# An unrolled attention stage with q, k and v laid out by the host, and a gate on the split x

## The chip, the cores and the metric

The kernel runs on one core of a Trainium2 chip, in one launch. The metric is the device time of that launch in microseconds, lower is better. All times here are of the kernel before; "the profiled execution" is one more execution of it, taken by the hardware profiler. Engines: PE is TensorE (PEld are its weight loads, which run beside its matmuls), DVE is VectorE, ACT is ScalarE, POOL is GpSimd, SP is SyncE, which issues most of the DMAs.

## What is computed

The reference, cut to what matters:

```python
# attention inside chunks of 64 tokens; q, k, v are [4, 8, 576, 64]
scores = (q_c @ k_c.T) / 8;  scores -= scores.max(-1)
attn = exp(scores) / (exp(scores).sum(-1) + 1e-9)
out = attn @ v_c                       # x = out as [2304 tokens, 512]
# mixture of experts, 8 experts, 512 -> 1024 -> 512
logits = x @ w_gate;  P = exp(logits - logits.max())
for _ in range(8):                     # balancing over rows and columns
    P /= P.sum(1) + 1e-9;  P /= P.sum(0) + 1e-9;  P *= N / E
out = sum over e of P[:, e:e+1] * (maximum(x @ w1[e], 0) @ w2[e])
# a last layer 512 -> 2048 -> 512
g = elu(out @ w_in);  result = g @ w_out
```

## The kernel before, in words

The 2304 tokens are 18 tiles of 128, in 6 blocks of 3 tiles. The experts and the last layer are 20 passes of 512 hidden columns each: a pass multiplies every block "up" (four groups of 12 matmuls with 384 columns, in groups f of 0 to 3) and "down" (three tiles of 12 matmuls with 512 columns). Each float32 operand of a pass is split in a rounded part and a rest (`x_hi`/`x_lo`, `w_hi`/`w_lo`, `h_hi`/`h_lo`), and three of the four products are taken.

The attention stage (blocks 0 to 5) runs together with pass 0: while block i's three tiles go through attention, the passes' work on block i-1 fills PE's gaps. What fills them is cut in `UNITS`: "up" f in two halves of 6 matmuls (`up_half`, L308) and "down" j in two halves of 6 (`down_tile`, L335), 14 units a block. The order is the hand-written list `STAGES` (L43), read by `block_schedule` (L55), the same on all engines; blocks 2 to 4 are a hardware loop, the others are unrolled. After block 5 the units of block 5 come alone (L442), then pass 1 begins (L448).

A tile's attention has six steps. **S0**: PE turns q and k by 4 transposes each into `ab_ps` (L370, L375), and ACT copies q (L519) and half of k (L522) out, DVE the other half of k (L661), into `k_wide`, which keeps zeros beside each chunk of k. **S1**: 8 float32 matmuls give the scores of all heads (L385; the trace has two records for each float32 matmul), DVE takes the row maximum (L665) and subtracts it (L668), ACT takes the exponential in two halves of 64 partitions (L530). **S2**: 8 transposes, one a head (L399), copied out by ACT (L536) and DVE (L673). **S3**: 8 matmuls with the turned exponentials as stationary operand and the values, with a column of ones beside them, as moving operand of 65 columns (L407); DVE adds to the sums (L677), takes reciprocals (L679) and multiplies (L682) to get `x_row`. **S4**: 4 transposes of x (L413), copied out by DVE (L687); ACT rounds it to `x_hi` (L540). **S5**: 4 float32 matmuls with 8 columns for the gate (L420), DVE copies the logits (L690) and makes `x_lo` (L694).

SP loads q, k and v of a tile with two DMAs each (L248) as its buffers come free. ACT issues the first 2 MB of weights (L566, L567), and splits them piece by piece (L506) in the last gaps of block 0, DVE making the rests (L646). POOL fills constants at the start (L276 to L284), takes the maximum over partitions once (L287) and scales the sum once after pass 1 (L295). The matmuls of the later passes are at L317 to L360.

## Time and profile before

| | us |
|---|---|
| median of 3 runs (lowest, highest) | 2164.53 (2163.47, 2165.15) |
| the profiled execution, its own time | 2163.2 |
| its span, first to last instruction | 2161.4 |
| PE busy in the span | 2130.3 |
| DVE, ACT, POOL busy | 823.4, 455.9, 22.4 |
| start to the first "up" of pass 0 | 57.91 |
| start to the first matmul of pass 1 | 259.31 |

The span is read as three stretches: the first block's attention alone, then five blocks of attention with pass 0 woven in (184.6 us together), then everything from pass 1 on, which the change does not edit. The granted clock is the share of full speed (2.4 GHz) that TensorE was given, 0.5 being 1.2 GHz.

### The profile page before, as it was taken

Reading aid. Unit: us, or ns where it says so; the run is one execution under the profiler, and the core shown is the slowest. Engines: PE = TensorE matmul, PEld = TensorE weight load, DVE = VectorE, ACT = ScalarE, POOL = GpSimd, SP = SyncE. Lnnn points to the kernel's source line nnn. Section 1 sums busy time; section 2 is a strip of 40 time slices with the busy share of each in tenths; the row PEclk is TensorE's granted clock in tenths of the full one; section 3 lists DMA queues with packets and bytes.
Section 4 is the critical chain, followed back from the end, with each engine's and each line's share of the span. In section 5 each row is a group of like instructions: output and inputs, shape, how many; then the busy total and the mean of one; then the engine's idle time right before and its main releaser. Section 6 shows DMA issues by size and latency. Waiting matters only on the chain.

```text
span 2161.4 us, 30934 instructions
## 1 busy us (share of the span) xinstructions
PE 2130.3 (99%) x11248; PEld 1937.2 (90%) x11248; DVE 823.4 (38%) x1439; ACT 455.9 (21%) x882; POOL 22.4 (1%) x29
## 2 busy tenths in 40 slices
PE   6999999999999999999999999999999999999999
PEld 5888899999999999999999999999999989999998
DVE  3444443332333233333333332333233345555544
ACT  3333311111111111111111111111111133223222
POOL 0000003000000000000000000000000000000000
PEclk8999999999999999999999999999999999999999
DMA  5223100000000100000000001000000000000001
GB/s 126 60 59 97 40 20 20 20 20 20 19 19 19 39 19 19 19 19 19 19 19 19 19 19 35 23 19 19 19 19 19 19 20 20 20 20 20 0 30 58
DMA packets 81304, 61.39 MB, mean 28 GB/s; under 512 B 58480, under 2 KB 58480, under 8 KB 81264
## 3 DMA queue, kind: packets, MB, share of 16 engines
q1 hardware_dynamic: 79680, 58.73, 9.0%
q10 hardware_dynamic: 1584, 2.11, 0.3%
q8 instruction: 26, 0.43, 0.1%
q14 instruction: 14, 0.11, 0.0%
HBM read 56.12 MB, written 4.72 MB: 28 GB/s over the span
## 4 chain that ended last, share of the span: by engine, by line
PE 96%; DVE 2%; issue 1%; ACT 1%; DMA 0%; ACTq 0%; SPq 0%; DVEq 0%; POOL 0%; POOLq 0%
PE down_ps L360 29%; PE up_ps L327 22%; PE ab_ps L360 14%; PE ab_ps L327 11%; PE cd_ps L327 11%; PE down_ps L346 2%; PE cd_ps L407 2%; PE up_ps L317 2%; PE cd_ps L385 1%; PE ab_ps L399 1%; PE ab_ps L413 1%; DVE row_max L665 1%; DVE x_row L682 0%; DVE soft L668 0%; PE cd_ps L480 0%
## 5 line engine op out<-in xcount | busy, mean ns | idle before, releaser
L513 ACT ACTIVATE h_hi<-up_ps 128x384 fp32r<-128x384 f32 x204 | 100.4, 492 | 1002.9 <-PE up_ps L327 955.9
L770 DVE SCALAR_TENSOR_TENSOR acc<-down_ps,route,acc 128x512 f32 x168 | 123.9, 751 | 424.0 <-PE down_ps L360 418.4
L651 DVE SCALAR_TENSOR_TENSOR h_lo<-up_ps,h_hi 128x384 fp32r<-128x384 f32 x204 | 113.8, 558 | 301.3 <-ACT h_hi L513 301.3
L360 PE MATMUL down_ps<-w_hi_b,h_lo 128*128 128x512 f32 x480 | 187.7, 391 | 0.0
L360 PE MATMUL down_ps<-w_lo_b,h_hi 128*128 128x512 f32 x480 | 187.4, 390 | 0.0
L360 PE MATMUL down_ps<-w_hi_b,h_hi 128*128 128x512 f32 x480 | 186.9, 389 | 0.0
L360 PE MATMUL down_ps<-w_hi_a,h_lo 128*128 128x512 f32 x432 | 169.0, 391 | 0.0
L360 PE MATMUL down_ps<-w_hi_a,h_hi 128*128 128x512 f32 x432 | 169.0, 391 | 0.0
L360 PE MATMUL down_ps<-w_lo_a,h_hi 128*128 128x512 f32 x432 | 168.7, 391 | 0.0
L327 PE MATMUL up_ps<-x_hi,w_lo_b 128*128 x480 | 161.1, 336 | 0.0
L327 PE MATMUL up_ps<-x_hi,w_hi_b 128*128 x480 | 161.0, 335 | 0.0
L327 PE MATMUL up_ps<-x_lo,w_hi_b 128*128 x480 | 160.8, 335 | 0.0
L327 PE MATMUL up_ps<-x_hi,w_hi_a 128*128 (+1 forms) x432 | 145.0, 336 | 1.7 <-DVE x_lo L805 1.7
L327 PE MATMUL up_ps<-x_hi,w_lo_a 128*128 (+1 forms) x432 | 145.0, 336 | 0.0
L327 PE MATMUL up_ps<-x_lo,w_hi_a 128*128 (+1 forms) x432 | 144.7, 335 | 0.0
L360 PEld LDWEIGHTS down_ps<-w_hi_b,h_lo 128*128 128x128 f32 x480 | 90.1, 188 | 18.8
L360 PEld LDWEIGHTS down_ps<-w_hi_b,h_hi 128*128 128x128 f32 x480 | 90.1, 188 | 17.2
L360 PEld LDWEIGHTS down_ps<-w_lo_b,h_hi 128*128 128x128 f32 x480 | 90.1, 188 | 17.1
L651 DVE SCALAR_TENSOR_TENSOR h_lo<-cd_ps,h_hi 128x384 fp32r<-128x384 f32 x90 | 50.2, 558 | 136.0 <-ACT h_hi L513 136.0
L651 DVE SCALAR_TENSOR_TENSOR h_lo<-ab_ps,h_hi 128x384 fp32r<-128x384 f32 x90 | 50.2, 558 | 132.2 <-ACT h_hi L513 132.2
L360 PEld LDWEIGHTS down_ps<-w_hi_a,h_lo 128*128 128x128 f32 x432 | 81.1, 188 | 17.0
L360 PEld LDWEIGHTS down_ps<-w_hi_a,h_hi 128*128 128x128 f32 x432 | 81.2, 188 | 15.3
(144 smaller groups left out, 4279.9 us busy)
## 6 DMA issues: line engine op xcount, KB each, us to landing
stage<-in_moe_w SPq DMA_DIRECT2D x30, 1024.0 KB, 5.0
q_raw<-in_q SPq DMA_DIRECT2D x36, 128.0 KB, 2.4
k_raw<-in_k SPq DMA_DIRECT2D x36, 128.0 KB, 2.8
v_raw<-in_v SPq DMA_DIRECT2D x36, 128.0 KB, 2.9
out<-acc SPq DMA_DIRECT2D x18, 256.0 KB, 2.0
stage<-in_moe_w_in SPq DMA_DIRECT2D x4, 1024.0 KB, 5.0
stage<-in_moe_w_out SPq DMA_DIRECT2D x4, 1024.0 KB, 5.1
stage<-in_moe_w ACTq DMA_DIRECT2D x2, 1024.0 KB, 8.8
```

The source lines that it names most:

```text
L317: mm = nc.tensor.matmul(up_ps[f % 2][:, 0:BLK], *terms[n], start=n == 0, stop=n == len(terms) - 1)
L327: mm = nc.tensor.matmul(hid_ps[f], w, x, start=n == 0, stop=n == len(terms) - 1)
L346: mm = nc.tensor.matmul(down_ps[j % 2][:, :], h, w, start=f == 0 and n == 0, stop=f == FT - 1 and n == 2)
L360: mm = nc.tensor.matmul(y_ps[j], h, w, start=f == 0 and n == 0, stop=f == FT - 1 and n == 2)
L385: mm = nc.tensor.matmul(scores[cs, 2 * m:2 * m + 2, :], q_t[:, m, cs], k_wide[:, m, c, :, :], start=True, stop=True)
L399: mm = nc.tensor.transpose(ab_ps[:, g, m * P:(m + 1) * P], e_wide[:, EH * g + m, :], ident[:, :])
L407: mm = nc.tensor.matmul(attn[:, g, m, :], e_t[:, EH * g + m, :], v_raw[j][:, EH * g + m, :], start=True, stop=True)
L413: mm = nc.tensor.transpose(ab_ps[:, 0, m * P:(m + 1) * P], x_row[:, 2 * m:2 * m + 2, :], ident[:, :])
L513: nc.scalar.activation(h_hi[:, f, :], bank, ACT.Relu).then_inc(h_hi_done, 1)
L651: nc.vector.scalar_tensor_tensor(h_lo[:, f, :], bank, 0.0, h_hi[:, f, :].bitcast(F32), ALU.max, ALU.subtract).then_inc(h_lo_done, 1)
L665: nc.vector.tensor_reduce(row_max[:, :], scores, AX_X, ALU.max).then_inc(max_done, 1)
L770: nc.vector.scalar_tensor_tensor(acc_tile(t), y_ps[j], route_flat[:, bass.ds(EXPERTS * t + expert, 1)], acc_tile(t), ALU.mult, ALU.add).th ...
```

## The change

The kernel's inputs q, k and v are laid out by the host before the launch (outside the metric): q and k transposed, tile by tile, so that a tile's q is 128 x 512 with head pairs on partitions and k is 64-row halves, and v by chunk and head pair. The turns of q and k (S0) and their copies are gone; SP loads q with one DMA and k and v with two each, straight into `q_t`, `k_wide` and `v_wide`, three buffers of each. The zeros of `k_wide` and `v_wide` are written by DVE (12 memsets of 64 x 512; `zero`). The softmax is normalised before the values: after one full-width exponential in place, DVE sums the rows (a new reduce), adds, takes reciprocals and multiplies into `x_row`, and PE turns two heads at once (4 transposes a tile for 8). The values are the stationary operand now, 64 columns each, and the turned weights move, 64 columns at a time: 16 matmuls a tile that write x already transposed. So x needs no turn and no copy, and ACT and DVE read `x_hi` and `x_lo` from PSUM. The gate is made once a block, from `x_hi` and `x_lo` with a padded 128-column stationary `gate_wide` (rounded weights in columns 0 to 7, rests in 8 to 15), copied by ACT, turned back by 3 transposes and added by DVE. POOL makes the rests of the first weights in place of DVE. Everything in the stage is unrolled.

On every engine the order (here tiles 6 to 8; "up1.1a" is half a of up 1 of block 1) is:

```
scores6 max6 shift6 down0.1b values5 x_hi5 x_lo5 down0.2a norm6 down0.2b up1.0a turn6 up1.0b
scores7 max7 shift7 up1.1a values6 x_hi6 x_lo6 gate1 gate_copy1 up1.1b norm7 up1.2a up1.2b turn7 up1.3a
scores8 max8 shift8 up1.3b values7 x_hi7 x_lo7 gate_turn1 logits1 down1.0a norm8 down1.0b down1.1a turn8
```

After tile 17 come gate5, then the 14 units of block 5 with `gate_turn(5)` behind the second, DVE's maximum of the logits there and its wait for POOL's `all_max` behind the fourth. The diff, cut to its core (new functions of PE, ACT and DVE stand as they are; of the removed ones see the listing above):

```diff
+def attention_schedule():
+    units = iter([(what, b, n, h) for b in range(BLOCKS - 1) for what, n, h in UNITS])
+    def some(count):
+        return [next(units) for _ in range(count)]
+    out = [("scores", 0), ("max", 0), ("shift", 0), ("scores", 1), ("max", 1), ("norm", 0), ("shift", 1), ("turn", 0),
+           ("scores", 2), ("max", 2), ("norm", 1), ("shift", 2), ("values", 0), ("x_hi", 0), ("x_lo", 0), ("turn", 1),
+           ("weights", 0), ("norm", 2), ("values", 1), ("x_hi", 1), ("x_lo", 1), ("turn", 2)]
+    for t in range(TPB, TILES):
+        b, where = divmod(t, TPB)
+        out += [("scores", t), ("max", t), ("shift", t)]
+        out += some(0 if b == 1 and where == 0 else 1)
+        out += [("values", t - 1), ("x_hi", t - 1), ("x_lo", t - 1)]
+        if where == 0:
+            out += [("weights", 1)] if b == 1 else some(1)
+            out += [("norm", t)] + some(1 if b == 1 else 2)
+        elif where == 1:
+            out += [("gate", b - 1), ("gate_copy", b - 1)] + some(1) + [("norm", t)] + some(2)
         else:
+            out += [("gate_turn", b - 1), ("logits", b - 1)] + some(1) + [("norm", t)] + some(2)
+        out += [("turn", t)] + some(0 if where == 2 else 1)
+    out += some(1) + [("values", TILES - 1), ("x_hi", TILES - 1), ("x_lo", TILES - 1)] + some(2)
+    assert next(units, None) is None
...
+        q_t = [at_arena(f"q_t{j}", [P, PAIRS, P]) for j in range(TPB)]
+        k_wide = [at_arena(f"k_wide{j}", [P, PAIRS, 2, 2, CHUNK]) for j in range(TPB)]
+        v_wide = [at_arena(f"v_wide{j}", [P, PAIRS, 2, 2, HD]) for j in range(TPB)]
+        e_t = at_arena("e_t", [P, PAIRS, P])
...
+        gate_wide = nc.alloc_sbuf_tensor_at("gate_wide", [P, KT, P], F32R, offset=acc_at + 4 * D * (TILES - 3))
+        gate_rows = nc.alloc_sbuf_tensor_at("gate_rows", [2 * EXPERTS, BLK], F32, offset=acc_at + 4 * D * (TILES - 2))
...
+        e_ps = ab_ps[:, 0, :]
+        x_ps = cd_ps[:, 1, :].rearrange("p (m n) -> p m n", m=KT)
+        gate_ps = ab_ps[:, 1, 0:BLK]
+        logit_ps = ab_ps[:, 1, BLK:BLK + 2 * TPB * EXPERTS].rearrange("p (j a e) -> p j a e", j=TPB, a=2)
...
+            def load_tile(t):
+                j = t % TPB
+                if t >= TPB:
+                    sp.wait_ge(scores_done, t - TPB + 1)
+                sp.dma_start(q_t[j][:, :, :], q[t, :, :, :]).then_inc(qk_loaded[j], 16)
+                for g in range(2):
+                    half = slice(HD * g, HD * g + HD)
+                    sp.dma_start(k_wide[j][half, :, :, g, :], k[t, half, :, :, :]).then_inc(qk_loaded[j], 16)
+                if t >= TPB:
+                    sp.wait_ge(values_done, t - TPB + 1)
+                for g in range(2):
+                    half = slice(CHUNK * g, CHUNK * g + CHUNK)
+                    sp.dma_start(v_wide[j][half, :, :, g, :], v[t, half, :, :, :]).then_inc(v_loaded[j], 16)
+            for t in range(TILES):
+                load_tile(t)
...
-            nc.gpsimd.memset(v_all[:, :, :, HD:VD], 1.0).then_inc(raw_free, TPB)
             nc.gpsimd.memset(ident[:, :], 0.0).then_inc(ident_zero, 1)
-            nc.gpsimd.memset(ones[:, :], 1.0).then_inc(const_ready, 1)
             pool.wait_ge(ident_zero, 1)
             nc.gpsimd.affine_select(out=ident[:, :], in_=ident[:, :], compare_op=ALU.not_equal, fill=1.0, base=0,
                                     pattern=[[-1, P]], channel_multiplier=1).then_inc(const_ready, 1)
-            nc.gpsimd.memset(e_wide[:, :, :], 0.0).then_inc(const_ready, 1)
-            nc.gpsimd.memset(k_wide[:, :, :, :, :], 0.0).then_inc(const_ready, 1)
+            nc.gpsimd.memset(gate_wide[:, :, :].bitcast(F32), 0.0).then_inc(gate_zero, 1)
+            nc.gpsimd.memset(ones[:, :], 1.0).then_inc(const_ready, 1)
+            pool.wait_ge(gate_hi_done, 1)
+            nc.gpsimd.tensor_tensor(gate_wide[:, :, EXPERTS:2 * EXPERTS], gate_w[:, :, :],
+                                    gate_wide[:, :, 0:EXPERTS].bitcast(F32), ALU.subtract).then_inc(gate_lo_done, 1)
+            for n in range(PIECES):
+                layer, kk = divmod(n, KT)
+                pool.wait_ge(w_hi_done, n + 1)
+                nc.gpsimd.tensor_tensor(w_lo[0][:, layer, kk, :], stage[:, layer, kk, :],
+                                        w_hi[0][:, layer, kk, :].bitcast(F32), ALU.subtract).then_inc(w_lo_done, 1)
...
+            def gate_rows_of(b):
+                pe.wait_ge(x_lo_done, TPB * (b + 1))
+                if b == 0:
+                    pe.wait_ge(gate_lo_done, 1)
+                else:
+                    pe.wait_ge(logits_done, b)
+                cols = slice(BLK * b, BLK * (b + 1))
+                for kk in range(KT):
+                    for x in (x_hi, x_lo):
+                        mm = nc.tensor.matmul(gate_ps, gate_wide[:, kk, :], x[:, kk, cols],
+                                              start=kk == 0 and x is x_hi, stop=kk == KT - 1 and x is x_lo)
+                mm.then_inc(gate_done, 1)
+            def gate_turn(b):
+                pe.wait_ge(gate_rows_done, b + 1)
+                for j in range(TPB):
+                    at = BLK + 2 * EXPERTS * j
+                    mm = nc.tensor.transpose(ab_ps[:, 1, at:at + 2 * EXPERTS], gate_rows[:, P * j:P * j + P],
+                                             ident[0:2 * EXPERTS, 0:2 * EXPERTS])
+                mm.then_inc(gate_turned, 1)
+            def attention(what, t):
+                j, r = t % TPB, t // TPB
+                if what == "scores":
+                    pe.wait_ge(qk_loaded[j], 48 * (r + 1))
+                    if t < TPB:
+                        pe.wait_ge(zeroed, 2 * (t + 1))
+                    if t > 0:
+                        pe.wait_ge(soft_done, t)
+                    for m in range(PAIRS):
                         for c in range(2):
                             cs = slice(CHUNK * c, CHUNK * c + CHUNK)
+                            mm = nc.tensor.matmul(scores[cs, 2 * m:2 * m + 2, :], q_t[j][:, m, cs],
+                                                  k_wide[j][:, m, c, :, :], start=True, stop=True)
                     mm.then_inc(scores_done, 1)
+                if what == "turn":
+                    if t == 0:
+                        pe.wait_ge(const_ready, 1)
                     else:
+                        pe.wait_ge(e_t_done, t)
+                    pe.wait_ge(norm_done, t + 1)
+                    for m in range(PAIRS):
                         mm = nc.tensor.transpose(ab_ps[:, 0, m * P:(m + 1) * P], x_row[:, 2 * m:2 * m + 2, :], ident[:, :])
+                    mm.then_inc(e_turned, 1)
+                if what == "values":
+                    pe.wait_ge(v_loaded[j], 32 * (r + 1))
+                    if t < TPB:
+                        pe.wait_ge(zeroed, 2 * (TPB + t + 1))
+                    pe.wait_ge(e_t_done, t + 1)
+                    if t > 0:
+                        pe.wait_ge(x_lo_done, t)
+                    for m in range(PAIRS):
+                        for c in range(2):
+                            for g in range(2):
+                                cs = slice(CHUNK * c, CHUNK * c + CHUNK)
+                                mm = nc.tensor.matmul(x_ps[HD * g:HD * g + HD, m, cs], v_wide[j][:, m, c, g, :],
+                                                      e_t[:, m, cs], start=True, stop=True)
+                    mm.then_inc(values_done, 1)
...
+            def gate_copy(b):
+                act.wait_ge(gate_done, b + 1)
+                if b > 0:
+                    act.wait_ge(gate_turned, b)
+                nc.scalar.activation(gate_rows[:, :], ab_ps[0:2 * EXPERTS, 1, 0:BLK], ACT.Copy).then_inc(gate_rows_done, 1)
+            def attention(what, t):
+                if what == "shift":
                     act.wait_ge(soft_done, t + 1)
+                    nc.scalar.activation(soft[:, :, :], soft[:, :, :], ACT.Exp, scale=SCALE).then_inc(exp_done, 1)
+                if what == "turn":
+                    act.wait_ge(e_turned, t + 1)
+                    if t > 0:
+                        act.wait_ge(values_done, t)
+                    nc.scalar.activation(e_t[:, :, :].rearrange("p a b -> p (a b)"), e_ps, ACT.Copy).then_inc(e_t_done, 1)
+                if what == "x_hi":
+                    act.wait_ge(values_done, t + 1)
+                    nc.scalar.activation(x_hi[:, :, P * t:P * t + P], x_ps, ACT.Copy).then_inc(x_hi_done, 1)
+            act.wait_ge(qk_loaded[0], 48)
             act.dma_start(stage[:, 0, :, :], w1_v[0, :, :, 0:FW]).then_inc(stage_loaded[0], 16)
             act.dma_start(stage[:, 1, :, :], w2_v[0, :, 0:KT, :]).then_inc(stage_loaded[1], 16)
+            act.dma_start(gate_w[:, :, :], w_gate.rearrange("(k p) e -> p k e", p=P)).then_inc(gate_loaded, 16)
...
+                elif what == "weights":
+                    split_weights(n, n, 0, range(KT))
+                    if n == 1:
+                        act.wait_ge(gate_loaded, 16)
+                        act.wait_ge(gate_zero, 1)
+                        nc.scalar.activation(gate_wide[:, :, 0:EXPERTS], gate_w[:, :, :], ACT.Copy).then_inc(gate_hi_done, 1)
...
+            def logits_of(b):
+                dve.wait_ge(gate_turned, b + 1)
+                nc.vector.tensor_copy(logit_sum[:, :, :], logit_ps[:, :, 0, :]).then_inc(logit_part_done, 1)
+                dve.wait_ge(logit_part_done, b + 1)
+                nc.vector.tensor_tensor(logits[:, TPB * b:TPB * (b + 1), :], logit_ps[:, :, 1, :], logit_sum[:, :, :],
+                                        ALU.add).then_inc(logits_done, 1)
+            def attention(what, t):
+                if what == "max":
                     dve.wait_ge(scores_done, t + 1)
                     nc.vector.tensor_reduce(row_max[:, :], scores, AX_X, ALU.max).then_inc(max_done, 1)
+                if what == "shift":
                     dve.wait_ge(max_done, t + 1)
+                    dve.wait_ge(norm_done, t)
                     nc.vector.tensor_tensor(soft[:, :, :], scores, row_max[:, :].unsqueeze(2).to_broadcast([P, HEADS, HD]),
                                             ALU.subtract).then_inc(soft_done, 1)
+                if what == "norm":
+                    dve.wait_ge(exp_done, t + 1)
+                    nc.vector.tensor_reduce(row_sum[:, :], soft[:, :, :], AX_X, ALU.add).then_inc(sum_done, 1)
+                    dve.wait_ge(sum_done, 3 * t + 1)
+                    nc.vector.tensor_scalar(row_den[:, :], row_sum[:, :], EPS, None, ALU.add).then_inc(sum_done, 1)
+                    dve.wait_ge(sum_done, 3 * t + 2)
+                    nc.vector.reciprocal(row_rec[:, :], row_den[:, :]).then_inc(sum_done, 1)
+                    dve.wait_ge(sum_done, 3 * t + 3)
+                    dve.wait_ge(e_turned, t)
+                    nc.vector.tensor_tensor(x_row[:, :, :], soft[:, :, :],
+                                            row_rec[:, :].unsqueeze(2).to_broadcast([P, HEADS, HD]), ALU.mult)\
+                        .then_inc(norm_done, 1)
...
+            def zero(wide):
+                nc.vector.memset(wide[0:HD, :, :, 1, :], 0.0).then_inc(zeroed, 1)
+                nc.vector.memset(wide[HD:P, :, :, 0, :], 0.0).then_inc(zeroed, 1)
+            for wide in (k_wide[0], k_wide[1], k_wide[2], v_wide[0]):
+                zero(wide)
+            for what, n, *unit in attention_schedule():
+                if (what, n) == ("norm", 0):
+                    zero(v_wide[1])
+                    zero(v_wide[2])
...
```

## Rows read from the trace of the kernel before

**Rows 1.** The page: the span, busy time, chain of waits by engine.
```profile
span 2161.4 us, 30934 instructions
...
PE 2130.3 (99%) x11248; PEld 1937.2 (90%) x11248; DVE 823.4 (38%) x1439; ACT 455.9 (21%) x882; POOL 22.4 (1%) x29
...
PE 96%; DVE 2%; issue 1%; ACT 1%; DMA 0%; ACTq 0%; SPq 0%; DVEq 0%; POOL 0%; POOLq 0%
```

**Rows 2.** Busy time by stretch (window: its length, busy us, then PEclk, DMA share, GB/s).
```profile
0.00:57.91 57.91, 39.76 (x213) 34.26 (x214) 22.73 (x41) 17.69 (x30) 2.67 (x10) 0.78 0.48 119
...
130.49:168.10 37.61, 35.95 (x266) 31.75 (x268) 17.72 (x34) 14.33 (x25) 0.00 (x0) 1.00 0.28 63
...
205.70:242.52 36.82, 34.83 (x257) 30.92 (x257) 17.84 (x36) 13.20 (x23) 0.00 (x0) 1.00 0.20 65
242.52:259.31 16.79, 16.79 (x85) 15.35 (x86) 8.37 (x18) 7.62 (x15) 0.38 (x1) 1.00 0.20 64
259.31:2161.40 1902.09, 1896.52 (x9665) 1730.56 (x9663) 706.01 (x1214) 360.47 (x715) 19.33 (x18) 1.00 0.06 22
```

**Rows 3.** Chain of waits in order of time (start us, us, what).
```profile
57.91 3.08 PE up_ps L317 x12
...
144.88 2.09 PE up_ps L317 x12
...
148.96 1.75 PE cd_ps L407 x16
...
155.93 4.11 PE down_ps L346 x18
```

**Rows 4.** Timeline of block 3 (start us, us, engine, line, out<-in, count).
```profile
130.41 0.85 PEld L385 LDWEIGHTS cd_ps<-k_wide,q_t 128*64 128x64 f32 x16
...
131.44 0.42 PEld L370 LDWEIGHTS ab_ps<-ident,q_raw 128*128 128x128 f32 x4 [0.17 <-issue]
...
139.67 0.17 DVE L677 TENSOR_SCALAR row_sum<-cd_ps 128x8 f32<-128x8 f32 x1 [2.10 <-PE cd_ps L407]
...
140.11 0.69 DVE L682 TENSOR_TENSOR x_row<-cd_ps,row_rec 128x512 f32<-128x512 f32 x1
...
140.40 0.34 PE L317 MATMUL up_ps<-x_hi,w_lo_a 128*128 x1
140.78 0.49 ACT L513 ACTIVATE h_hi<-up_ps 128x384 fp32r<-128x384 f32 x1 [3.73 <-PE up_ps L317]
140.85 0.42 PEld L413 LDWEIGHTS ab_ps<-ident,x_row 128*128 128x128 f32 x4 [0.43 <-DVE x_row L682]
...
141.30 0.56 DVE L651 SCALAR_TENSOR_TENSOR h_lo<-up_ps,h_hi 128x384 fp32r<-128x384 f32 x1 [0.50 <-ACT h_hi L513]
141.44 0.85 PEld L385 LDWEIGHTS cd_ps<-k_wide,q_t 128*64 128x64 f32 x16 [0.17 <-issue]
```

**Rows 5.** Timeline of the start (same columns).
```profile
1.47 0.95 POOL L283 MEMSET e_wide<- 128x1024 f32 x1
...
5.77 1.09 PE L370 MATMUL ab_ps<-ident,q_raw 128*128 128x128 f32 x4 [5.77 <-DMA k_raw<-in_k]
...
9.81 1.60 PEld L385 LDWEIGHTS cd_ps<-k_wide,q_t 128*64 128x64 f32 x16 [2.50 <-ACT q_t L519]
9.84 1.97 PE L385 MATMUL cd_ps<-k_wide,q_t 128*64 128x128 f32 x16 [2.13 <-ACT k_wide L522]
11.74 0.72 PEld L370 LDWEIGHTS ab_ps<-ident,q_raw 128*128 128x128 f32 x4 [0.33 <-DMA k_raw<-in_k]
...
43.16 1.67 ACT L506 ACTIVATE w_hi_a<-stage 128x512 fp32r<-128x512 f32 x3
```

**Rows 6.** Groups of instructions, 0 to 400 us (count | busy us, mean ns | idle before).
```profile
L530 ACT ACTIVATE e_wide<-soft 64x512 f32<-64x512 f32 x36 | 22.7, 630 | 32.8 <-DVE soft L668 32.4
...
L295 POOL TENSOR_TENSOR acc<-acc,route x18 | 19.3, 1074 | 115.0 <-issue 114.3
...
L668 DVE TENSOR_TENSOR soft<-cd_ps,row_max 128x512 f32<-128x512 f32 x18 | 12.4, 692 | 1.5
```

More of the change, by code:

```diff
@@ L401, in attention @@
-                if stage_name == "S3":
-                    pe.wait_ge(v_loaded[j], 32 * (i + 1))
-                    pe.wait_ge(soft_done, t + 1)
-                    for g, ready in ((0, e_t_lo), (1, e_t_hi)):
-                        pe.wait_ge(ready, t + 1)
-                        for m in range(EH):
-                            mm = nc.tensor.matmul(attn[:, g, m, :], e_t[:, EH * g + m, :], v_raw[j][:, EH * g + m, :],
-                                                  start=True, stop=True)
-                    mm.then_inc(attn_done, 1)
@@ L424, in block_of_work @@
-            def block_of_work(i, schedule):
-                for what, n, half in schedule:
-                    if what == "up":
-                        if n == 0 and half == 0:
-                            pe.wait_ge(x_lo_done, TPB * i)
-                        up_half(i - 1, n, half)
-                    elif what == "down":
-                        down_tile(i - 1, 0, 0, n, half)
-                    elif what != "split":
-                        attention(what, TPB * i + n, n, i)
-            pe.wait_ge(const_ready, 4)
@@ new lines, in _ @@
+            for what, n, *unit in attention_schedule():
+                if what == "up":
+                    if unit == [0, 0]:
+                        pe.wait_ge(x_lo_done, TPB * (n + 1))
+                    up_half(n, *unit)
+                elif what == "down":
+                    down_tile(n, 0, 0, *unit)
+                elif what == "gate":
+                    gate_rows_of(n)
+                elif what == "gate_turn":
+                    gate_turn(n)
+                else:
+                    attention(what, n)
@@ L448, in _ @@
+            gate_rows_of(BLOCKS - 1)
+            for n, (what, f, half) in enumerate(UNITS):
+                if what == "up":
+                    up_half(BLOCKS - 1, f, half)
+                else:
+                    down_tile(BLOCKS - 1, 0, 0, f, half)
+                if n == 1:
+                    gate_turn(BLOCKS - 1)
+            pe.wait_ge(const_ready, 2)
+            pe.wait_ge(x_lo_done, TILES)
+            pe.wait_ge(e_t_done, TILES)
+            pe.wait_ge(logits_done, BLOCKS)
             with pe.Fori(0, 2) as jj:
@@ new lines, in _ @@
+            gate_copy(BLOCKS - 1)
+            act.wait_ge(values_done, TILES)
+            for n, (what, f, half) in enumerate(UNITS):
+                if half == 1 and what == "up":
+                    hidden_hi(BLOCKS - 1, f, up_ps[f % 2][:, 0:BLK])
+                if half == 1 and what == "down":
+                    acc_out(BLOCKS - 1, f)
+                if n == 5:
+                    act.wait_ge(neg_max_done, 1)
+                    nc.scalar.activation(route_flat, logits_flat, ACT.Exp, bias=neg_max[:, 0:1]).then_inc(balance, 1)
@@ new lines, in _ @@
+            for wide in (k_wide[0], k_wide[1], k_wide[2], v_wide[0]):
+                zero(wide)
+            for what, n, *unit in attention_schedule():
+                if (what, n) == ("norm", 0):
+                    zero(v_wide[1])
+                    zero(v_wide[2])
+                if what == "up":
+                    if unit[1] == 1:
+                        hidden_lo(n, unit[0], up_ps[unit[0] % 2][:, 0:BLK])
+                elif what == "logits":
+                    logits_of(n)
+                elif what not in ("down", "weights", "gate", "gate_copy", "gate_turn"):
+                    attention(what, n)
@@ new lines, in _ @@
+            for n, (what, f, half) in enumerate(UNITS):
+                if half == 1 and what == "up":
+                    hidden_lo(BLOCKS - 1, f, up_ps[f % 2][:, 0:BLK])
+                if n == 1:
+                    logits_of(BLOCKS - 1)
+                    dve.wait_ge(logits_done, BLOCKS)
+                    nc.vector.tensor_reduce(part_max[:, :], logits_flat, AX_X, ALU.max).then_inc(part_max_done, 1)
+                if n == 3:
+                    dve.wait_ge(all_max_done, 1)
+                    nc.vector.tensor_scalar(neg_max[:, :], all_max[:, :], -1.0, None, ALU.mult).then_inc(neg_max_done, 1)
```

275 lines of the change are left out of this document (46 added, 229 removed), and 3 rows, old and new, of the table STAGES.

## The prediction

> **What bounds the kernel now.** I read the page first: PE is busy for 2130.3 of 2161.4 us, and the chain that ended last is 96% PE's [rows 1]. So a change pays where it takes PE work away, or PE waiting. Busy time by stretch says where [rows 2]. From 259.31 us on the kernel runs passes 1 to 19, 1902.1 us with PE idle for 5.6; no edit reaches them, and I leave them as they are. The attention stage before them has two parts. Up to 57.91 us block 0 goes through attention with nothing to fill the gaps: PE works 39.8 us of 57.9, and the clock granted is 0.78 on average. From 57.91 to 242.52 us five blocks follow with pass 0 woven in, 37.61 us each in the middle (168.10 less 130.49), PE 35.95 busy, clock 1.00. The 14 units of block 5 alone take 16.79. So attention costs a block 37.61 - 16.79 = 20.82 us of PE's path, 6.94 a tile, almost all of it PE work. DVE and ACT are busy for 17.7 and 14.3 us of such a block. PE is the bound, and its order is fixed by hand.
>
> The chain gives the prices of PE work at full clock [rows 3]: 12 "up" matmuls 2.09 us (174 ns each), 18 "down" 4.11 (228 ns), the values' 16 records 1.75 (109 ns).
>
> **A tile's PE work after.** The scores stay: 16 weight loads in 0.85 us (53 ns a record), and 0.17 us before and behind them in which no weight load starts, where 128*64 changes to 128*128 [rows 4]. That is 0.85 + 2 x 0.17 = 1.19, with the last load's tail 1.22 us. The turn of `x_row` is one group of 4 transposes like L413's: 0.42, taken as 0.43 [rows 4]. The turns of q, k and x and half of those of the exponentials are gone.
>
> The values in their new form (64 stationary columns, 64 moving, 32 records a tile) don't occur. What bounds a record there isn't plain. The nearest row is the scores' 53 ns: the same 64 stationary columns, the same alternation between two column groups, but 128 moving columns [rows 4]. If loads set that pace, the values keep it; if the moving columns did, it halves to 27. From above: 109 ns, the old values' [rows 3], which load 128 columns. I take 53: 32 x 0.053 = 1.71, plus 2 x 0.17 for the two changes of form, 2.05 us. Bounds: 32 x 0.027 + 0.34 = 1.2, and 32 x 0.109 + 0.34 = 3.83 us. So the values get no cheaper than the old 1.75 although they turn x for nothing.
>
> The idle 0.17 beside each 128*64 group is what the Trainium skill (TensorEngine Tiling (Array Packing), Key Properties) calls a drain on a change of tiling mode; it speaks against this change, which doubles such changes, and the trace agrees with 0.17 us for one. The same section lets different tiles load and multiply in parallel, which is the 27 ns case; no row here separates it.
>
> The gate, once a block: 8 matmuls of 384 columns at 174 ns [rows 3], 1.39, and 3 transposes like L413's, 0.33: 1.72. Between half of and double the transposes' price this moves the sum by under 3 us, since there are only 18.
>
> Per block: 16.79 + 3 x (1.22 + 0.43 + 2.05) + 1.72 = 29.6 us of PE work for 37.6.
>
> **What PE waits for then.** In the steady order I follow each tile's `norm` to its `turn`. DVE's operations of 128x512 take 0.69 [rows 6]; reads from SBUF are not shown for the new row sum, but they can't be far: I use 0.69 + 0.03, and from L677's start to L682's end 1.13 [rows 4], so `norm` is 1.85. Tile 6: scores end at 1.0 us of its slot, maximum and shift at 2.6, exponential at 3.3 (0.63 for 64 partitions [rows 6]; for 128 I take the same). `norm6` starts behind `x_lo5`, at about 5.9, and ends at 7.75; `turn6` comes at 8.3 in PE's order. No wait. Tile 8: 7.8 against 8.6. No wait. Tile 7: `norm7` stands behind the rest of up1.1 on DVE. That matmul's result is there 0.17 after its slot, then 0.04 + 0.49 + 0.03 + 0.56 [rows 4], then 1.85: 3.15 us, while PE has only two halves of "up", 2.1. PE waits 1.1 us, once a block. Everything else (copy of `e_t`, x_lo before the next values, gate copies, three buffers of loads, SP's order q, k, v) has at least 1 us to spare by the same reckoning. The DVE adds for logits (0.4) lie beside "down".
>
> **The start.** Most of block 0 is a chain through three engines at the low clock: scores take 1.97 us there for 1.05 [rows 5]. Loads: the first matmul came at 5.77 after four DMA issues for q and k; now three, so 5.2. scores0 to 7.2, max and shift to 8.65. scores1 needs tile 1's k, which in the old run had landed only at 11.7, behind 2 MB of weights [rows 5]; it is issued an operation earlier twice over, so I take 10.0, and 12.0 at the end. max1 12.7. Then DVE clears `v_wide` 1 and 2: four memsets of 512 elements; POOL took 0.95 for 1024, so 0.5 each (bounds 0.2 and 0.69), 14.7. norm0 16.6, shift1 17.3, scores2 19.3, and values0 at the low clock 3.6 to 22.9. max2, norm1, shift2 to 22.65, exp2 23.3, x_hi0, the copy of turn 1 to 24.55, values1 from 24.7 to 28.3, turn2 29.05, scores3 31.0, values2 34.6.
>
> Here I expect a wait that the change brings. The first "up" needs four of the eight rests of the weights, and these are POOL's now. But POOL stands before them at the wait for `gate_hi_done`, which ACT gives only after it has rounded all eight pieces, and ACT does pieces 4 to 7 behind `x_hi2`. So: x_hi2 35.3, four pieces at 0.57 [rows 5] 37.6, the gate's copy 37.85, its rest on POOL 38.1, and four subtractions like L295's at 1.07 [rows 6] 42.4. The first "up" starts at 42.4 us, for 57.91 before. Without this order it could start when x_lo2 is there, at 36.0; so 6.4 us of the gain is left there. Behind POOL queue only the later rests, due at "down" 0, in time. PE has then idled for nearly 8 us, so it begins at 1.2 GHz; the same point before cost 3.08 us for 12 matmuls instead of 2.09 [rows 3], and I allow 2 us.
>
> **Sum.** From 42.4: five blocks' units 5 x 16.79 = 83.95; scores 4 to 17, 14 x 1.22 = 17.1; turns 3 to 17, 15 x 0.43 = 6.45; values 3 to 17, 15 x 2.05 = 30.75; five gates 5 x 1.72 = 8.6; waits 5 x 1.1 = 5.5; together 152.3. The low clock 2. Gate 5 and block 5's units 1.72 + 16.79 = 18.5, with `all_max` (0.38 busy on POOL [rows 2]) hidden by a unit of "up". Pass 1 starts at 42.4 + 152.3 + 2 + 18.5 = 215.2, for 259.3 before: 44.1 us less. The profiled execution took 2163.2, so 2119.1; the median of the runs shown stands 1.3 above it, so **2120.4**. Fetching the longer unrolled code I cost at nothing: blocks 0, 1 and 5 were unrolled already and show no wait for it; if that cover fails, it shows as issue time on PE.
>
> **Rivals.** (1) *The values run at half the pace's price*, 27 ns a record: 15 x 0.85 less, and about 3 us less at the low clock at the start, 16 in all: 2105. For it, no load of two column groups is seen to collide; against it, 64 columns loaded in half of the time of 128 is just what 53 and 109 ns are. Chance 0.15. (2) *The records are dearer*, between 53 and 109 ns: at 109, 15 x 1.78 + 7 = 34 more, 2155; the middle gives 2137. For it, two records a matmul with only 64 moving columns leave little to hide a start behind, a form that no row has. Chance 0.2. Beside this stands the Trainium skill (TensorE: Matmul & The Clock Gate, Back-to-back issue gap), which gives some 81 ns for a sustained pair of load and matmul at 128 columns. By that rule the values would take 32 x 0.081 + 0.34 = 2.9 us and the kernel 2136 (an estimate); the scores' 53 ns in this trace speak against it. (3) *PE waits more than once a block*: DVE has six operations of 0.69 a tile, and if each tile waits as tile 7 does, 10 x 1.1 = 11 more, 2131; against it, 0.6 and 0.8 us of slack at tiles 6 and 8. Or the start is better, with a clock that rises early as at 25 us before: 4 less. Chance 0.08, inside my range. (4) *Slower*: each change of column group waits until the record before it is through. Place: the `g` loop of `values`, PE. In the old trace a matmul record lasts some 270 ns from start to end; at 270 a record the values take 8.7 us, 15 x 6.65 + 15 = 115 more, 2235. It decides from the point where 15 warm tiles and about 4 warm tiles' worth at the start eat 44 us: 2.3 us a tile, 125 ns a record. Against it, the scores alternate groups at 53. The low clock for the whole stage, PE with gaps of 1.1 us, would do the same; against it, clock 1.00 with PE 95% busy in each old block, while the new block has 29.6 of 30.7. Chance 0.05 together.
>
> **The numbers.** My forecast, 2112 to 2129, has 0.5; with the rivals this fills the sum, but for 0.02 that the change does nothing measurable. The range, 2104 to 2146, takes in rival 1's price, though about a third of its chance lies below it (a smaller pace still), the dearer values up to some 90 ns a record, and rival 3; left out are that 0.05, a fifth to a third of rival 2, rival 4 and the 0.02, together under 0.2. Faster 0.93, same 0.02, slower 0.05. A difference of 0.2%, 4.3 us, is about what a measurement of this kernel tells from none.
>
> **What would show it.** Right: first "up" near 42 us, with PE idle behind values2 and a wait for POOL's `w_lo_a`; 32 value records in about 1.9 us; blocks of 30.7 us; a wait for `x_row` of DVE once a block, about 1.1; pass 1 from 215 us, and 1902 us behind it. Wrong: value records far from 53 ns, a DVE wait in every tile, a clock under 1 between 50 and 210 us, or a longer stretch behind pass 1.

## The result, and the profile after

The changed kernel takes 2109.5 us (median of 4 runs, 2107.24 to 2111.19) for 2164.0 in the same comparison: ratio 0.9747, interval 0.973 to 0.9764. Measured once more beside later experiments it took 2109.7 (ratio 0.9749, 0.9734 to 0.9764). The forecast was 2120.4 with a range of 2104 to 2146, so sign and range held, and the gain is 54.5 us where 44.1 had been worked out. The narrower 2112 to 2129, which had a chance of 0.5, did not hold.

The page of the changed kernel: span, busy time, chain.

```profile
span 2108.1 us, 30180 instructions
PE 2067.6 (98%) x11170; PEld 1877.8 (89%) x11170; DVE 799.0 (38%) x1401; ACT 426.2 (20%) x835; POOL 31.5 (1%) x36
PE 97%; DVE 1%; DMA 0%; ACT 0%; POOL 0%; issue 0%; SPq 0%; DVEq 0%; ACTq 0%
```

PE's busy time fell by 62.7 us and the span by 53.3; beside [rows 1], POOL does 9 us more. Busy time by stretch of the changed kernel, columns as in [rows 2]:

```profile
0.00:45.42 45.42, 15.49 (x172) 13.29 (x173) 20.15 (x39) 11.20 (x20) 6.65 (x14) 0.92 0.67 162
...
105.18:133.45 28.27, 27.32 (x252) 23.26 (x252) 13.50 (x27) 9.38 (x17) 0.00 (x0) 1.00 0.33 84
...
187.53:205.97 18.44, 18.44 (x96) 16.72 (x96) 8.73 (x20) 8.70 (x17) 0.70 (x1) 1.00 0.17 58
205.97:2108.10 1902.13, 1896.48 (x9665) 1730.65 (x9663) 705.68 (x1214) 360.52 (x715) 19.33 (x18) 1.00 0.06 22
```

Against [rows 2]: the stretch behind pass 1 is what it was (1902.1 both). The start went from 57.91 to 45.42, 12.5 us less. The five blocks went from 184.6 (57.91 to 242.52) to 142.1 (45.42 to 187.53), 42.5 less; one in the middle takes 28.27 for 37.61. The last stretch has the gate in it and takes 1.65 more. 12.5 + 42.5 - 1.65 is the 53.3 of the span.

Inside a block, the chain of waits of the changed kernel, in order of time (start, us, what). The slot of the block's second tile:

```profile
105.18 1.05 PE up_ps L322 x6
106.23 1.02 PE cd_ps L402 x16
107.25 1.26 PE up_ps L322 x6
108.51 1.08 PE cd_ps L425 x32
109.59 1.59 PE ab_ps L379 x8
111.18 1.05 PE up_ps L322 x6
...
112.26 0.50 ACT h_hi L523
...
112.78 0.56 DVE h_lo L654
113.34 0.60 DVE row_sum L678
...
114.41 0.70 DVE x_row L685
...
115.25 0.63 PE ab_ps L412 x4
```

L402 are the scores, L425 the values, L379 the gate, L412 the turn of `x_row`. Two things are to be seen. The 32 value records take 1.08 us and make what follows 0.2 longer (1.59 where eight such matmuls are 1.39), 1.29 in all, where the sum had 2.05. And the chain leaves PE once a block, through h_hi, h_lo and norm to the turn, as worked out. The weight loads of both forms (timeline):

```profile
106.16 0.85 PEld L402 LDWEIGHTS cd_ps<-k_wide,q_t 128*64 128x64 f32 x16 [0.25 <-issue]
108.44 1.01 PEld L425 LDWEIGHTS cd_ps<-e_t,v_wide 128*64 128x64 f32 x32 [0.26 <-issue]
115.22 0.42 PEld L412 LDWEIGHTS ab_ps<-ident,x_row 128*128 128x128 f32 x4 [1.23 <-issue]
```

One load lasts 138 ns, so 31 starts share 1.01 - 0.14: 28 ns from record to record, for 48 in the scores (15 starts in 0.85 - 0.14). The prediction's 53 for the scores is the 0.85 divided by 16, with the last load's tail in it. The start, same kernel, timeline:

```profile
5.16 1.98 PE L402 MATMUL cd_ps<-k_wide,q_t 128*64 128x128 f32 x16 [5.16 <-DMA k_wide<-in_k]
...
14.85 1.97 PE L402 MATMUL cd_ps<-k_wide,q_t 128*64 128x128 f32 x16 [7.71 <-DMA k_wide<-in_k]
...
24.63 1.94 PEld L425 LDWEIGHTS cd_ps<-e_t,v_wide 128*64 128x64 f32 x32
...
37.84 0.69 DVE L691 TENSOR_TENSOR x_lo<-cd_ps,x_hi 128x512 fp32r<-128x512 f32 x1 [1.18 <-ACT x_hi L547]
...
40.08 0.32 POOL L282 TENSOR_TENSOR gate_wide<-gate_w,gate_wide 128x32 fp32r<-128x32 f32 x1 [38.00 <-ACT gate_wide L565]
40.36 9.86 POOL L288 TENSOR_TENSOR w_lo_a<-stage,w_hi_a 128x512 fp32r<-128x512 f32 x8
...
45.42 0.66 PE L322 MATMUL up_ps<-x_hi,w_hi_a 128*128 128x384 f32 x1 [9.30 <-POOL w_lo_a L288]
```

The wait for POOL is there, 9.3 us of idle PE, and tile 1's k landed at 14.8 us, 5 later than taken. Up to 38 us the granted clock reads 1.00 in these rows, yet the scores take 1.97 us for the 1.09 of a block's; PE idles from 36.1 us on, and the granted clock is 0.50 from 39 to 48 us and 1.00 again from 49. What PE waits for in the whole changed kernel (the three largest of five lines; us in total, times, longest):

```profile
PE cd_ps L402 <- DMA k_wide<-in_k: 12.9, 2, 7.7
PE ab_ps L412 <- DVE x_row L685: 11.1, 7, 5.2
PE up_ps L322 <- POOL w_lo_a L288: 9.3, 1, 9.3
...
```

### The profile page after: what moved, and what is told of

The parts are those of the page before. It is cut to its first block, busy times and chain, and to the rows that moved or that the text cites. A ratio compares the mean times of both kernels' runs of the same rounds, so it can differ in the third digit from the quotient of the medians.

```text
span 2108.1 us, 30180 instructions
## 1 busy us (share of the span) xinstructions
PE 2067.6 (98%) x11170; PEld 1877.8 (89%) x11170; DVE 799.0 (38%) x1401; ACT 426.2 (20%) x835; POOL 31.5 (1%) x36
## 4 chain that ended last, share of the span: by engine, by line
PE 97%; DVE 1%; DMA 0%; ACT 0%; POOL 0%; issue 0%; SPq 0%; DVEq 0%; ACTq 0%
PE down_ps L365 30%; PE up_ps L332 23%; PE ab_ps L365 15%; PE ab_ps L332 11%; PE cd_ps L332 11%; PE down_ps L351 2%; PE up_ps L322 2%; PE cd_ps L402 1%; PE cd_ps L425 1%; PE ab_ps L412 0%; DMA k_wide<-in_k 0%; PE ab_ps L379 0%; PE cd_ps L490 0%; DVE x_row L685 0%; POOL w_lo_a L288 0%
```

## The experiments

All start from the changed kernel; where an edit adds lines, line numbers shift by one or two. "Pass 1" is the start of its first matmul in the profiled execution (205.8 us in the changed kernel, 205.5 in its repeat). Medians come from the runs beside the kernel before, which stood at 2163.5 to 2163.6 in these comparisons.

**POOL's order.**

```diff
-            pool.wait_ge(gate_hi_done, 1)
-            nc.gpsimd.tensor_tensor(gate_wide[:, :, EXPERTS:2 * EXPERTS], gate_w[:, :, :],
-                                    gate_wide[:, :, 0:EXPERTS].bitcast(F32), ALU.subtract).then_inc(gate_lo_done, 1)
             for n in range(PIECES):
...
+            pool.wait_ge(gate_hi_done, 1)
+            nc.gpsimd.tensor_tensor(gate_wide[:, :, EXPERTS:2 * EXPERTS], gate_w[:, :, :],
+                                    gate_wide[:, :, 0:EXPERTS].bitcast(F32), ALU.subtract).then_inc(gate_lo_done, 1)
```

> Edit: POOL makes the eight rests of the first weights before it waits for gate_hi_done and makes the gate's rest. Theory (PE's 9.3 us of idle ahead of the first 'up' is POOL standing at the gate's wait): the first four rests are ready at about 35.5 us, the first 'up' then waits for x_lo of tile 2 only and starts at 38.7 instead of 45.4 us; pass 1 starts at about 199 instead of 206.0, the whole takes about 2103. Rival (POOL's subtractions themselves are too slow, or something else behind them is late): the first 'up' moves by less than 2 us, and the time stays within 2 us of 2109.5.

2104.8 us (2104.22 to 2105.89; ratio 0.973, 0.9713 to 0.9746). Its timeline:

```profile
20.48 1.97 PE L402 MATMUL cd_ps<-k_wide,q_t 128*64 128x128 f32 x16 [0.60 <-DMA k_wide<-in_k]
...
27.98 5.41 POOL L285 TENSOR_TENSOR w_lo_a<-stage,w_hi_a 128x512 fp32r<-128x512 f32 x4 [25.90 <-ACT w_hi_a L516]
28.24 1.05 DVE L680 TENSOR_SCALAR row_den<-row_sum 128x8 f32<-128x8 f32 x1
...
29.56 1.47 DVE L685 TENSOR_TENSOR x_row<-soft,row_rec 128x512 f32<-128x512 f32 x1
...
37.56 0.45 PE L322 MATMUL up_ps<-x_hi,w_hi_a 128*128 128x384 f32 x1 [2.00 <-DVE x_lo L691]
```

The wait for POOL is gone, the first "up" waits for x_lo as the theory has it, and starts at 37.56, 7.9 us earlier. Not all of that is the edit: in this execution tile 1's scores began at 11.6 us, 3.3 earlier than in the changed kernel's. What the order alone is worth is read below, together with the later weights, which fix that landing. Pass 1 came at 200.6, 5.2 earlier only. The lines name one cost not reckoned with: beside POOL, DVE's addition of 128x8 took 1.05 us and the multiplication 1.47, against 0.17 and 0.69 in the changed kernel. So part of the gain may have been given back there, which the later runs take up.

**The weights' DMA later.**

```diff
-            act.wait_ge(qk_loaded[0], 48)
-            act.dma_start(stage[:, 0, :, :], w1_v[0, :, :, 0:FW]).then_inc(stage_loaded[0], 16)
-            act.dma_start(stage[:, 1, :, :], w2_v[0, :, 0:KT, :]).then_inc(stage_loaded[1], 16)
-            act.dma_start(gate_w[:, :, :], w_gate.rearrange("(k p) e -> p k e", p=P)).then_inc(gate_loaded, 16)
             for what, n, *unit in attention_schedule():
...
+                if (what, n) == ("shift", 0):
+                    act.wait_ge(qk_loaded[1], 48)
+                    act.dma_start(stage[:, 0, :, :], w1_v[0, :, :, 0:FW]).then_inc(stage_loaded[0], 16)
+                    act.dma_start(stage[:, 1, :, :], w2_v[0, :, 0:KT, :]).then_inc(stage_loaded[1], 16)
+                    act.dma_start(gate_w[:, :, :], w_gate.rearrange("(k p) e -> p k e", p=P)).then_inc(gate_loaded, 16)
```

> Edit: ACT issues the first 2 MB of weights only when tile 1's q and k have landed, behind the first exponential. Theory (tile 1's k landed at 14.85 us because the 2 MB of weights share the DMA engines with it): it lands by 9.5 us, scores1 starts there, and pass 1 starts 4 to 6 us earlier, at 200 to 202 us; the whole takes about 2104.5. Rival (the new k transfers with their 256-byte pieces are slow by themselves): scores1 still starts at 13 to 15 us and nothing is won; the weights may then even come late.

2104.7 us (2104.40 to 2105.05; ratio 0.9728, 0.9712 to 0.9744), pass 1 at 200.7.

```profile
8.96 1.98 PE L402 MATMUL cd_ps<-k_wide,q_t 128*64 128x128 f32 x16 [1.61 <-DMA k_wide<-in_k]
...
39.63 0.66 PE L322 MATMUL up_ps<-x_hi,w_hi_a 128*128 128x384 f32 x1 [8.69 <-POOL w_lo_a L288]
```

scores1 starts at 8.96 for 14.85: the 2 MB of weights, not the new transfers' form, had held up tile 1's k. In seven other profiles with the early weights tile 1's scores started between 11.6 and 14.6 us, in the three others with the later weights at 9.2. The four runs lie within 0.65 us, those of the changed kernel within 3.95. Whether this race of transfers makes the spread between runs is not shown: the repeat of the changed kernel, with the early weights too, spread by 1.47 only.

**norm ahead of h_lo in the second tile.**

```diff
-            out += [("gate", b - 1), ("gate_copy", b - 1)] + some(1) + [("norm", t)] + some(2)
+            out += [("gate", b - 1), ("gate_copy", b - 1), ("norm", t)] + some(3)
```

> Edit: in the second tile of each block DVE does the normalisation ahead of the h_lo of up 1, not behind it. Theory (PE waits 0.94 us a block at the turn because norm stands behind h_lo): the wait for x_row goes in all five blocks, a block takes 27.3 instead of 28.27 us, pass 1 starts at about 201.3, the whole takes about 2105. Rival (DVE is short in that slot anyway, the wait moves to the next 'up' or the next tile): blocks shrink by less than 0.3 us.

2102.9 us (2100.32 to 2103.96; ratio 0.9719, 0.9702 to 0.9735). The chain at the gates of blocks 3 and 4:

```profile
105.50 1.59 PE ab_ps L379 x8
132.64 1.59 PE ab_ps L379 x8
```

A block takes 27.14 us for 28.27, 1.13 less, and none of the five waits for `x_row` is left. Of the 7.7 us by which pass 1 came earlier (198.1), 5.6 are these; the first "up" came 2.3 earlier, with tile 1's k, which landed at 12.4 in this execution.

**The values, one column group after the other.**

```diff
-                    for m in range(PAIRS):
-                        for c in range(2):
-                            for g in range(2):
+                    for g in range(2):
+                        for m in range(PAIRS):
+                            for c in range(2):
```

> Edit: the 16 value matmuls of a tile in another order, first the eight of column group 0, then the eight of group 1; same matmuls. Theory (a record costs 27 to 31 ns because loads of the two column groups overlap when they alternate): without alternation a record costs about 53 ns, the values 1.7 to 1.9 us a tile instead of 1.08, a block 30.2 to 30.7 instead of 28.27, pass 1 starts at 216 to 219 us. Rival (64 moving columns set the pace, whatever the group): nothing changes, 206 us.

One execution, 2119.7 us; pass 1 at 215.7. The chain, and a load group of the timeline:

```profile
113.37 1.61 PE ab_ps L379 x8
143.92 1.61 PE ab_ps L379 x8
```

```profile
111.47 1.76 PEld L425 LDWEIGHTS cd_ps<-e_t,v_wide 128*64 128x64 f32 x32 [0.25 <-issue]
```

The same 32 records take 1.83 us for 1.08: (1.76 - 0.14)/31 is 52 ns, twice 28. A block takes 30.55, and 3 x 0.75 is the difference. So 53 ns is right for a values' record that follows one of its own group, and the order of the loops halves it.

**The scores, one column group after the other.**

```diff
-                    for m in range(PAIRS):
-                        for c in range(2):
+                    for c in range(2):
+                        for m in range(PAIRS):
```

> Edit: the 8 score matmuls of a tile in another order, the four of column group 0 first, then the four of group 1. The values at 55 ns a record in one group may be paced by 64 stationary columns or by 64 moving ones; here 64 stationary columns meet 128 moving ones. Theory (in one group the moving columns set the pace, two groups share it): 107 ns a record, the scores take 1.8 us instead of 1.02, a block 2.4 us more. Rival (the weight load sets it, 53 ns for 64 columns): the scores stay within 0.15 us of 1.02 and the block at 28.3 us.

One execution, 2119.4 us, pass 1 at 215.3:

```profile
102.10 1.34 PEld L402 LDWEIGHTS cd_ps<-k_wide,q_t 128*64 128x64 f32 x16 [0.17 <-issue]
```

Neither theory holds: (1.34 - 0.14)/15 is 80 ns, between the 53 of "only the load counts" and the 107 of "only the columns count"; the scores take 1.51 us for 1.02, a block 29.74. Within one group, 64 more moving columns cost 28 ns, alternating 20 (48 against 28).

**The gate twice.**

```diff
-                for kk in range(KT):
+                for kk in list(range(KT)) * 2:
```

> Edit: the 8 gate matmuls of a block are done twice, with the same result. Theory (PE's order is the path in every slot; what PE does more comes out one for one): a block 1.39 us longer, 29.66, and pass 1 about 8.3 us later with respect to the first 'up'. Rival (the slot has room because the turn behind it waits for DVE anyway): less than 0.5 us a block.

```profile
111.81 2.97 PE ab_ps L379 x16
...
141.48 2.97 PE ab_ps L379 x16
```

A block takes 29.67, 1.40 more; from the first "up" to pass 1 it is 169.9 us for 161.6 in the repeat of the changed kernel (43.92 to 205.52), 8.3 for 8.4 of added matmuls. The whole took 2117.7. PE's work is the path, one for one, also in the slot that ends in a wait.

**DVE's row sum twice.**

```diff
+                    nc.vector.tensor_reduce(row_spare[:, :], soft[:, :, :], AX_X, ALU.add)
                     nc.vector.tensor_reduce(row_sum[:, :], soft[:, :, :], AX_X, ALU.add).then_inc(sum_done, 1)
```

> Edit: in the changed kernel DVE sums each tile's exponentials twice, 0.69 us more a tile. Theory (only the second tile of a block waits for DVE; the others have slack): a block takes 0.7 us more, about 29.0 instead of 28.27, all of it in the wait for x_row of that tile. Rival (DVE sets the pace of every tile): 2.1 us more a block, 30.3. Rival (DVE nowhere on the path): no change in the blocks.

The chain at two blocks' gates:

```profile
140.90 1.59 PE ab_ps L380 x8
...
169.82 1.59 PE ab_ps L380 x8
```

28.92 us a block, 0.65 more, though DVE does 2.0 us more. The other two tiles have the slack that the prediction gave them. One execution, 2114.3.

**POOL's order and the later weights together.**

> Edit: the edits of the first two experiments together, so that POOL's order is seen without the changing landing of tile 1's k. Theory (both waits are in series on PE's path, the landing first, POOL later): scores1 at 9 us, x_lo of tile 2 at 33 to 34 us, and the first 'up' there instead of 39.6 as with the later weights alone; pass 1 at about 195.5 instead of 200.8; the whole about 2099.5. Rival (POOL's subtractions, now beside the start's chain, hold up DVE so much that it takes back what the order gives; with POOL's order alone two multiplications of DVE took 1.5 us instead of 0.69): pass 1 not before 199 us.

2101.7 us (ratio 0.9713, 0.9698 to 0.9728), pass 1 at 197.7, first "up" at 34.54. Both theories hold half: the first "up" is 5.1 us earlier than with the later weights alone, pass 1 only 2.9. Six matmuls behind the first "up" PE now waits for norm 3 (timeline):

```profile
37.57 1.08 PE L412 MATMUL ab_ps<-ident,x_row 128*128 128x128 f32 x4 [1.69 <-DVE x_row L686]
```

In the chain the additions and multiplications of norm 2 and 3 last 1.06, 1.48, 0.58 and 1.48 us; in norm 3 that is 1.2 us more than usual, out of the 1.7 of this wait.

**All four edits**: POOL's order, the later weights, norm ahead of h_lo, and the two clears of value buffers moved to ahead of scores1 on DVE. The last one's part of the diff:

```diff
-                if (what, n) == ("norm", 0):
+                if (what, n) == ("scores", 1):
                     zero(v_wide[1])
                     zero(v_wide[2])
```

> Edit: POOL's order, the later weights, norm ahead of h_lo in the second tile, and the clearing of the two value buffers moved ahead of the wait for scores1. Theory (the four are in series on PE's path): against the later weights alone the first 'up' comes 7 to 8 us earlier, at about 32 us, blocks take 27.14 us, pass 1 starts at 187 to 188, the whole takes about 2091. Rival (they cover each other in part: DVE, slowed by POOL, becomes the chain of the start and x_lo of tile 2 is what is late): pass 1 at 190 us or later, the whole 2094 or more.

2094.2 us (2093.72 to 2094.82; ratio 0.9679, 0.9666 to 0.9692). The first "up" came at 32.08 as the theory said, pass 1 at 189.8, nearly where the rival had it: of what was taken away, 2 us came back behind the first "up". The same DVE lines are the suspects (timeline):

```profile
22.50 5.40 POOL L285 TENSOR_TENSOR w_lo_a<-stage,w_hi_a 128x512 fp32r<-128x512 f32 x4 [20.42 <-ACT w_hi_a L516]
22.77 1.04 DVE L681 TENSOR_SCALAR row_den<-row_sum 128x8 f32<-128x8 f32 x1
...
24.08 1.47 DVE L686 TENSOR_TENSOR x_row<-soft,row_rec 128x512 f32<-128x512 f32 x1
```

**POOL behind the norms.**

```diff
             for n in range(PIECES):
                 layer, kk = divmod(n, KT)
+                if kk == 0:
+                    pool.wait_ge(norm_done, TPB + layer)
```

> Edit: the four edits together, and POOL starts the rests of the first weights only when DVE's norm of tile 2 is done, those of the second only behind the norm of tile 3. Theory (two DVE operations of each of these norms took 0.4 to 0.9 us longer because POOL's subtractions ran beside them): all DVE operations of norm 2 and 3 take their usual 0.17 and 0.69 us, the first 'up' comes about 1.5 us earlier and pass 1 starts at 187.5 to 188.5 instead of 189.9; the whole takes about 2092.5. Rival (the long operations have another reason, as the copies that ACT makes at the same time): they stay at 1.0 and 1.5 us, and POOL's later start makes the first 'up' late.

2089.5 us (2088.90 to 2091.08; ratio 0.9658, 0.9645 to 0.9671), pass 1 at 184.9.

```profile
23.76 0.17 DVE L683 TENSOR_SCALAR row_den<-row_sum 128x8 f32<-128x8 f32 x1
...
24.20 0.69 DVE L688 TENSOR_TENSOR x_row<-soft,row_rec 128x512 f32<-128x512 f32 x1
24.98 4.96 POOL L287 TENSOR_TENSOR w_lo_a<-stage,w_hi_a 128x512 fp32r<-128x512 f32 x4 [22.90 <-ACT w_hi_a L518]
...
30.77 0.44 PE L324 MATMUL up_ps<-x_hi,w_hi_a 128*128 128x384 f32 x1 [2.42 <-DVE x_lo L694]
```

DVE's operations are back at 0.17 and 0.69, and POOL's own four take 4.96 for 5.40. The first "up" is 1.3 us earlier, as expected; pass 1 is 4.9 earlier, 3 more than expected. Busy time by stretch shows the rest, first with the four edits, then with POOL behind the norms (window, PE, PEld, DVE, ACT, POOL, then the granted clock):

```profile
22.00:30.00 8.00, 6.28 (x82) 5.82 (x84) 5.28 (x8) 3.17 (x6) 5.40 (x4) 0.50 0.75 169
30.00:38.00 8.00, 4.62 (x24) 3.75 (x20) 3.68 (x6) 3.91 (x8) 5.64 (x5) 0.71 0.39 98
```

```profile
22.00:30.00 8.00, 5.07 (x84) 4.48 (x84) 4.43 (x8) 5.29 (x11) 4.96 (x4) 0.79 0.81 185
30.00:38.00 8.00, 6.44 (x71) 5.37 (x72) 4.25 (x8) 4.19 (x9) 5.22 (x5) 1.00 0.47 110
```

PE had its 2.4 GHz from about 26 us on and kept it, while in the other the granted clock fell back to 0.50 at about 34.3 us, when PE sat idle for norm 3, and the scores at 38 us still took 1.98. From the turn behind the first "up" to the next values it is 6.7 us there and 3.9 here: that is the 3 us, and it is the clock's, while the shorter norms give about 1.2 beside the 1.3 of the first "up". The granted clock fell to 0.50 in all three profiles with POOL beside norm 3 (POOL's order alone, with the later weights, all four edits: at about 38.5, 36.0 and 34.3 us), where PE waited 1.5 to 1.7 us for `x_row`; here the wait is 0.54 and the clock stayed. But in the first of them it fell while PE was still in the six matmuls ahead of that wait, so the reason stays open. The five runs within 2.2 us speak for the edit. This version is the fastest measured, 74 us under the kernel before.

**The changed kernel again.**

> The changed kernel as it is, once more, beside the two others on the same chip. Every theory expects 2107 to 2111 us, with scores1 starting anywhere from 12 to 15 us as tile 1's k lands.

2109.7 us (2108.81 to 2110.28); tile 1's scores started at 13.97, the first "up" at 43.92, pass 1 at 205.5.

## Why the prediction was right, and where it was off

- **What bounds it**: right. PE's order is the path: doubled gates came out one for one, and DVE's added 0.69 us a tile only in the tile that waits. Everything behind pass 1 stayed at 1902.1.
- **The scores, the turn, the gate**: right. 1.02 us and 0.2 behind it, for 1.22 taken; 0.44 for 0.43; 1.39 and 0.29 for 1.72. The longer unrolled code, taken at nothing, shows no issue time in PE's chain (0%).
- **The values: the step that was off.** "The nearest row is the scores' 53 ns ... I take 53 ... 2.05 us." It measured 1.29 with its changes of form, and 15 x 0.76 = 11.4 us is more than the whole miss. By the prediction's own list a record far from 53 ns is a sign of being wrong, and so are, in size, the 28.3 us a block for 30.7 and pass 1 at 205.8 for 215. Rival 1 was right in price (27 ns, 1.2 us), and had a chance of 0.15. My case against it, that 64 columns in half of the time of 128 is just what 53 and 109 are, compared a row that alternates column groups with one that doesn't. The two experiments on loop order show 52 ns for values of one group in a row and 28 alternating, 80 and 48 for scores. Of rival 1's two grounds the first, that two groups' work overlaps, is borne out; the second, that the moving columns alone set the pace, falls (80, not 107). Within a group 64 more moving columns cost 28 ns, which leaves 24 for the rest of a record. That this rest is its load is argued only: no run varied the stationary columns, and the old values, with 128 of them and 65 moving, took 109. Two groups share a record's time almost in halves (28 for 52) or less well; why the scores' 80 becomes 48 and not 40 stays open.
- **The rules named beside it**: the drain on a change of tiling mode in the Trainium skill (TensorEngine Tiling (Array Packing), Key Properties) agrees with 0.17 to 0.26 us without a load beside each form. Its statement there that different tiles load and multiply in parallel agrees with 28 against 52 ns. The 81 ns of the Trainium skill (TensorE: Matmul & The Clock Gate, Back-to-back issue gap) is for 128 moving columns, and the prediction set it on values that have 64: the scores, which have 128, came at 80 ns within one group and 48 alternating, the values at 52 and 28. The Trainium skill (TensorE: Matmul & The Clock Gate, Part 3, The mechanism) has loads overlap running matmuls only where row groups differ; here all records use all rows, only the column group differs, and alternation about halves the pace, so the measurement speaks against that rule for this form.
- **The first wait**: right in cause and nearly in size. PE idled 9.3 us at the first "up" for 7.8 worked out; without the order it fell to 2.0. POOL's subtraction took 1.26 us a piece where 1.07 had been taken from another operation, and the gate's rest 0.32 for 0.25. Of the 6.4 us said to be left there, 5.1 came back at the first "up", but only 2.9 at pass 1.
- **The start**: 45.4 for 42.4, 3.0 later. Tile 1's k landed 4.9 us late ("so I take 10.0"): the old 11.7 had been read as an upper end, but ACT's weights are now issued first, at 5.14 and 5.62, with the gate's transfer behind them and not ahead, beside this k's own issues (4.56 to 5.77). Two groups of values at the start's slow pace, 1.9 to 2.0 us for 3.6, and the third at 1.1 gave part back. The four clears took 2.4 us for 2.0. So x_hi of tile 2 came at 37.2 for 35.3, and POOL's four pieces added 0.8. That two misses of several us nearly cancel here is luck.
- **The wait in the second tile**: right, 0.94 us for 1.1 (2.1 us of PE beside 3.0 of ACT and DVE), and right that the others have slack.
- **The sum**: values -11.4, start +3.0, waits -0.8, clock -0.3 (the first three groups behind 45.42 took 1.7 more than in later blocks, for 2 allowed), and the median stands 0.35 under the profiled execution where 1.3 above had been carried over, -1.65. Together -11.2, against 2109.5 - 2120.4 = -10.9.

## What to carry to other kernels

With 64-column stationary operands, order the matmuls so that successive ones go to different column groups; here that halved 32 records a tile, and a price for a new form must come from a row with the same alternation and both sizes. Where work moves to an idle engine, read what stands ahead of it in that engine's queue, and which operations of a neighbour it will run beside: POOL's order cost 5 us at the first "up" and 3 at pass 1, and POOL's place beside DVE's chain another 5, of which nearly 3 were the clock's. Small transfers that the first steps need should land before megabytes that are first read 25 us later are issued.

## What was not expected of the hardware

- Beside POOL's 128x512 subtractions, DVE's addition on 128x8 took up to 1.06 us for 0.17, and its multiplication with two SBUF operands 1.47 for 0.69, while the row sum and the operations that read PSUM kept 0.68. Starting POOL behind them put all back. The Trainium skill (SBUF — State Buffer, SBUF: two separate sides) calls the pair of ports that the two engines share an exclusive lock held for a whole instruction; the multiplication, which has two SBUF operands beside a POOL operation that reads SBUF, agrees with it. The addition has one SBUF operand; the Trainium skill names DVE's 2-port modes there as the other case, and no run here shows which mode it ran in.
- Loads of 256-byte pieces beside 2 MB of weights landed 9 us after issue (14.8 against 4.6 to 5.8), and at 9.0 us without them.
- The values' form follows TensorE's clock. With the later weights a group of 32 loads ran while the granted clock was 0.50: 1.82 us, (1.82 - 0.23)/31 = 51 ns from one to the next with 0.23 for the last, against 28 at 1.00. At the start of the changed kernel the same loads took 1.94 us, 55 ns, though the granted clock reads 1.00 there; that the engine ran at the lower level in that stretch is seen from the lengths alone.
